# Attention and two feed-forward layers in one kernel: where ScalarE rounds keys and queries, and where VectorE sums, in the first 18 slots

## The reference

```python
scores = scale * np.matmul(q, k.transpose(0, 1, 3, 2))
kth = np.partition(scores, -top_k, axis=-1)[..., -top_k:-top_k + 1]
scores = np.where(scores >= kth, scores, -1000000000.0)
attn = np.exp(scores - np.max(scores, axis=-1, keepdims=True))
attn = attn / (np.sum(attn, axis=-1, keepdims=True) + 1e-09)
x = np.matmul(attn, v)                    # then heads side by side: 2304 x 512
h = x @ w_in                              # layer 1
g = np.where(h >= 1, h, np.where(h <= -1, 0.0, (h + 1) ** 2 / 4.0))
y = g @ w_out
h2 = np.maximum(y @ w_in2, 0.0)           # layer 2
out = h2 * h2 @ w_out2
```

## Time and profile before

| | |
|---|---|
| median of 3 runs | 1221.03 us |
| the profiled execution | 1220.98 us, of which the span from first to last instruction is 1219.2 us |
| mean granted TensorE clock | 0.982 |
| busy | PE 96%, PEld 89%, DVE 68%, ACT 64%, POOL 61% |

### The profile page before, as it was taken

How to read it: one execution, slowest core, us unless ns; L and a number is a source line. 1 busy time by engine, 2 the same in 40 slices (tenths; PEclk the granted TensorE clock), 3 DMA queues, 4 the chain that set the end, 5 groups by cost and what they waited for, 6 DMA issues and landing times.

```text
span 1219.2 us, 22952 instructions
## 1 busy us (share of the span) xinstructions
PE 1174.0 (96%) x8120; PEld 1089.9 (89%) x8120; DVE 833.0 (68%) x1847; ACT 784.0 (64%) x1704; POOL 740.3 (61%) x589
## 2 busy tenths in 40 slices
PE   5878999999999999999999999999999999999998
PEld 3777899999889999999999999998999888998887
DVE  7999999999988799999999987878830211110000
ACT  7887777787656767767676665666554544653343
POOL 6777887888877677677776766666742222222222
PEclk9957999999999999999999999999999999999999
DMA  6777897678869923433458831567449400870000
GB/s 252 266 267 252 282 360 295 251 268 315 302 253 393 379 75 109 147 121 112 140 208 297 294 112 41 130 173 183 109 160 361 167 1 1 338 318 1 1 35 18
DMA packets 93377, 237.34 MB, mean 195 GB/s; under 512 B 10320, under 2 KB 45136, under 8 KB 80976
## 3 DMA queue, kind: packets, MB, share of 16 engines
q1 hardware_dynamic: 93104, 235.62, 54.9%
q10 hardware_dynamic: 160, 0.26, 0.1%
HBM read 164.02 MB, written 71.83 MB: 193 GB/s over the span
## 4 chain that ended last, share of the span: by engine, by line
PE 74%; DVE 9%; POOL 8%; ACT 4%; issue 3%; DMA 1%; SPq 0%; ACTq 0%; POOLq 0%; DVEq 0%
PE h_ps L700 22%; PE y_ps L728 11%; PE y_ps L734 10%; PE pv_ps L659 6%; PE score_ps L700 6%; DVE top L1086 5%; PE tr_ps L632 4%; DVE rest L1088 4%; PE score_ps L605 3%; POOL s_sb L1270 3%; POOL prob L1275 2%; POOL kq_lo L1253 2%; PE y_ps L720 2%; PE y_ps L723 2%; PE tr_ps L720 2%
## 5 line engine op out<-in xcount | busy, mean ns | idle before, releaser
L700 PE MATMUL h_ps<-xt_ks,w_in 128*128 128x256 f32 (+1 forms) x2628 | 384.5, 296 | 2.3 <-ACT rg L961 1.6
L700 PEld LDWEIGHTS h_ps<-xt_ks,w_in 128*128 128x128 f32 x2628 | 342.1, 191 | 12.8 <-ACT rg L961 2.0
L1288 POOL TENSOR_TENSOR g_lo<-rg,g_hi 128x256 fp32r<-128x256 f32 x224 | 169.4, 756 | 270.4 <-ACT g_hi L974 153.6
L1086 DVE MAX8 top<-rest 128x8 f32<-128x576 f32 x432 | 305.1, 746 | 0.4
L1270 POOL TENSOR_SCALAR s_sb<-s_sb,top 128x576 f32<-128x576 f32 x126 | 221.5, 1758 | 31.3 <-DVE top L1086 31.3
L1088 DVE MATCH_REPLACE8 rest<-top,rest 128x576 f32<-128x576 f32 x288 | 211.5, 741 | 0.0
L1275 POOL TENSOR_TENSOR prob<-s_sb,prob 128x576 f32<-128x576 f32 x128 | 182.9, 1431 | 16.3 <-ACT s_sb L856 3.5
L728 PE MATMUL y_ps<-g_hi,w_out 128*128 128x256 f32 x896 | 181.4, 285 | 0.6 <-POOL g_lo L1288 0.5
L734 PE MATMUL y_ps<-w_out,g_hi 128*128 128x512 f32 x448 | 158.5, 395 | 1.0 <-ACT moves L935 0.8
L728 PEld LDWEIGHTS y_ps<-g_hi,w_out 128*128 128x128 f32 x896 | 147.5, 191 | 2.1 <-POOL g_lo L1288 1.0
L659 PE MATMUL pv_ps<-v_sb,pt 128*128 128x65 f32 x1024 | 133.6, 288 | 0.0
(11 more groups left out here) (117 smaller groups left out, 1821.8 us busy)
## 6 DMA issues: line engine op xcount, KB each, us to landing
w_in<-w_scratch SPq DMA_DIRECT2D x32, 1024.0 KB, 7.1
w_out<-w_scratch SPq DMA_DIRECT2D x32, 1024.0 KB, 8.4
xt_ks<-kq_scratch SPq DMA_DIRECT2D x30, 576.0 KB, 7.2
w_scratch<-w_in SPq DMA_DIRECT2D x16, 1024.0 KB, 7.2
w_scratch<-w_out SPq DMA_DIRECT2D x16, 1024.0 KB, 6.7
v_sb<-in_vv_dram SPq DMA_DIRECT2D x48, 325.0 KB, 6.1
qs_g<-kq_scratch SPq DMA_DIRECT2D x120, 128.0 KB, 4.3
moves<-in_w_dram SPq DMA_DIRECT2D x27, 512.0 KB, 5.9
```

Source lines behind the costliest of these rows:

```text
L700: last = pe.matmul(h_bank(k), wi[:, f // 2, w, m, cols], x_part(k, x, m), start=(m == 0 and n == 0), stop=(m == KT - 1 and n == 2))
L1086: dve.max(best, src[:, :]).then_inc(rank_step, 1)
L1288: pool.tensor_tensor(lo_of(k), u_of(k), hi_of(k).bitcast(F32), ALU.subtract).then_inc(g_lo_done, 1)
```

## The change

In slots 1, 3, 5 and 7 ScalarE's rounding of a preparation (`split_new`) goes from ahead of `exponentiate(n, 1)` to behind `copy_shared(n - 1)`, ahead of `split_ahead(n)`. In slots 10, 12, 14 and 16 VectorE's `add_to_total` goes from ahead of `rank(n, 0, 2)` to between the two ranks of op 2, `invert_total` from between these to between the two ranks of op 3, and ScalarE's `scale_pv` from ahead of `copy_scores(n + 1, 0)` to behind `copy_main(n - 1, 0)`. No operation is added or dropped.

```diff
@@ ScalarE, slot(n)
-                if n in SINGLE:
+                if n in SINGLE and n not in PREP_SLOT:
                     scale_pv(n - 2)
                 if nxt:
                     copy_scores(n + 1, 0)
...
                 copy_at(q)
                 if n in PREP_SLOT and n in SINGLE:
+                    scale_pv(n - 2)
                     hi_at(q)
-                if n in SINGLE or q < UP_POS[0]:
+                if n in SINGLE:
                     split_new(n)
                 if here:
                     exponentiate(n, 1)
...
                     copy_shared(n - 1)
                 copy_at(q + 1)
                 hi_at(q + 1)
+                if n < SINGLE[0]:
+                    split_new(n)
                 split_ahead(n)
@@ VectorE, slot(n)
-                    if past and op == 2 + behind and n not in SUMMED:
+                    if past and op == 2 + behind and n not in SUMMED and not (n in SINGLE and n in PREP_SLOT):
                         add_to_total(n - 2)
...
                         rank(n, 0, op)
-                        if op == 2 and n in SINGLE:
+                        if op == 2 and n in SINGLE and n in PREP_SLOT:
+                            add_to_total(n - 2)
+                        if op == (3 if n in PREP_SLOT else 2) and n in SINGLE:
                             invert_total(n - 2)
                         rank(n, 1, op)
```

## The result

| | before | after |
|---|---|---|
| median of the runs side by side, us | 1221.07 (1220.47 to 1224.06, 6 runs) | 1231.26 (1230.34 to 1233.01, 6 runs) |
| profiled execution, us | 1220.98 | 1230.34 |
| its span, us | 1219.2 | 1228.5 |
| VectorE's rank (10, 0) starts, us | 107.25 | 115.62 |
| VectorE's rank (18, 0) starts, us | 193.45 | 202.97 |

The ratio is 1.0082, 95% interval 1.0069 to 1.0096: 8.4 to 11.7 us slower. The forecast was +6.4, with 1230.0 as the top of the range; the medians show +10.2, the two profiled executions +9.3. The direction is right, the size is too small.

A forecast was written before the change was run, and what follows sets the result against it. VectorE's ranking sets the pace up to 107.2 us, and TensorE, busy from 193.4 us, can't absorb early delays. Terms of 6.3 and 0.3 gave +6.6, taken as +6.4: 1227.4 us, range 1222.5 to 1230.0.

The forecast's parts named there:

- Part 1: Rounding (kq_hi) later on ScalarE in slots 1, 3, 5, 7: late masks and loads delay VectorE, growing to +6.3 us.
- T: Start of ScalarE's rounding in slots 1, 3, 5, 7: 27.17, 49.9, 72.7 and 93.4 us.
- T + 6.4: GpSimd: mask(n, 0) can't start earlier than 6.4 us after the rounding's start, behind split_kq and the weight split.
- the steps from T to T: Transposes, scores, copies and times_v between two roundings: 20.7 us with no late load, over VectorE's 19.6 for two slots.
- Slot 9 has no rounding, so it stops there: Slot 9: the delay of VectorE's ranks grows no further than the +6.3 us at rank (9, 1).
- part 2: Sum, reciprocal and scale_pv later in slots 10, 12, 14, 16: slot 10 0, then +0.1 us three times, +0.3.
- The loads: SP's queue: queries of slots 4 and 6 land late, 5.3 us after issue, 0.8 us more delay in slot 3.
- Rival A: Loads of queries land early, so slots 4 and 6 don't wait: rank (9, 1) at 101.6, total 1224.7 us; chance 0.20.
- Rival C: TensorE's clock stays low in slots 8 and 9, 1.6 us a slot: +8 to +8.5, 1229.3 us; chance 0.10.
- after denser work: TensorE: times_v's products take 1.90 us at 98.07, following denser work, against 3.52 at the low clock level.
- That chain had 0.20 us of wait plus some 0.09 of wake-up: ScalarE's chain to g_hi, slot 14: room of 0.3 us against scale_pv's 0.4, so it ends 0.1 us later.
- The sum: Whole kernel: 6.3 + 0.3 = +6.6 us, taken as +6.4, giving 1227.4 us.

The follow-up runs named there:

- the swap: Late rounding in slots 1, 3, 5, 7, plus GpSimd's weight split ahead of the preparation's in slots 0 to 9, against the kernel before: 1220.63 us (-0.7), ratio 0.9994.
- the sum a pair later: Late rounding in slots 1, 3, 5, 7, plus slot 9's sum and reciprocal a pair of ranks later, against the kernel before: 1227.89 us (+6.4), ratio 1.0052.
- slots 3, 5 and 7 late alone: Kernel before with only the rounding of slots 3, 5 and 7 late: 1228.07 us (+6.3), ratio 1.0056.
- part 2 alone: Kernel before with only sum, reciprocal and scale_pv later in slots 10, 12, 14, 16: 1222.49 us (+1.1), ratio 1.0010.
- four pieces: Later sum, reciprocal and scale_pv, with GpSimd's preparation split in four instructions in slots 10, 12, 14, 16, against the kernel before: 1221.94 us (+0.6), ratio 1.0003.
- the rounding's idle place: Changed kernel with weight split first in slots 0 to 9 and rounding behind exponentiate(n, 0) in slots 10 to 16, against before: 1219.24 us (-2.6), ratio 0.9978.
- the two parts alone: Kernel before with only the late rounding of slots 1, 3, 5, 7: 1228.91 us (+7.6); with only the changes in slots 10, 12, 14, 16: 1222.49 us (+1.1).
- only the sum later: Kernel before with only the sum of slots 10, 12, 14, 16 half a pair of ranks later: 1221.91 us (+0.4), ratio 1.0003.
- the two last ones: Changed kernel, weight split first, rounding in ScalarE's idle place in slots 10 to 16: 1219.24 us; the same with slots 1 to 7 rounded early: 1218.64 us.

## Why the prediction was right or wrong

**Part 1's path: right.** Each step of it can be laid beside the profile after:

| | forecast | after |
|---|---|---|
| start T of the rounding, slots 1, 3, 5, 7 | 27.17, 49.9, 72.7, 93.4 | 27.29, 50.01, 73.02, 93.82 |
| mask(1, 0), mask(3, 0) start | 33.55, T + 6.4 = 56.3 | 33.64, 56.36 |
| rank (3, 1) | 39.04 | 39.28 |
| rank (5, 1) | 61.0 | 61.28 |
| rank (7, 1) | 83.8 | 84.29 |
| rank (9, 1) | 104.5 | 105.09 |

The start of the mask at T + 6.4 hit within 0.1 us, and the swap shows that this queue on GpSimd is the cause: with the weight split out of it part 1 costs nothing. How the loss divides between masks and loads is open. Each later rank is 0.2 to 0.6 us behind the forecast, since the steps from T to T were summed slightly short; rank (9, 1) is 6.9 us later than before, not 6.3. (The 49.9 of slot 3 is a slip: 47.6 + 1.4 + 0.8 is 49.8.)

**Part 1's end: "Slot 9 has no rounding, so it stops there" failed.** VectorE's sum reads slot 9's delay too. It waits 1.30 us for the product, and rank (10, 0) is 8.4 us late where I had stopped at 6.3. I had followed only the tiles that the rank reads, and had looked at the product only in part 2's slots. In slots 0 to 8 the sum stands a pair of ranks later in VectorE's order (behind = 2) and is covered; slot 9 is the first of the closer setting, and it receives the whole delay. With the sum a pair later the wait is gone. It also took the clock's low level on that one product, which with slots 3, 5 and 7 late alone was at the high one and made nobody wait.

**The loads: right.** They land late, with 5.4 us from the issue of the second load of queries (62.01 + 0.62) to TensorE's start at 68.05, where the earlier trace rows give 5.3. Rival A, early landing, would have given 101.6 for rank (9, 1). For a transfer of this size the estimate from the Trainium skill, DMA: Bandwidth & Descriptors, "Anatomy of one DMA", is 2.3 us. For these loads, behind six others, the traces don't agree with it.

**Rival C, the clock: its size came out, in part by luck.** I had written +8 to +8.5 for low clock in slots 8 and 9. Rank (10, 0) came at +8.37. Slot 8's product ran at the high level (1.90 us; 3.52 before, at 89.23), slot 9's at the low one (3.52; 1.90 before), and without the second there would have been no wait of 1.30. That is the clock's part; C's sum needs about 2 us of it, and the rest was made up by the steps from T to T. It was the rival nearest to the result, and I had given it 0.10. The rule of the Trainium skill that I cited with it, that the clock follows how busy TensorE has been, is neither borne out nor refuted by these runs. From 60 to 113 us TensorE is busy 39.28 us at a clock of 0.56 in after and 42.91 us at 0.63 before, which would agree. But "after denser work" was a misreading: in the 7 us ahead of the short product at 98.07 TensorE was busy 5.75 us with 27 matmuls, in the 7 ahead of the long one at 79.24 it was busy 6.27 with 26. And the same program up to slot 9's sum had its high level on slot 8's product in two kernels' executions and on slot 7's in a third.

**Part 2: "That chain had 0.20 us of wait plus some 0.09 of wake-up" failed.** The direction is right, and so is the first step (scale_pv's time leaves an idle place of ScalarE and comes ahead of the rounding). The size was 0.1 for a pair and is 0.38 to 0.43, and the path behind the rounding was another. I took the idle time in front of g_hi, 0.20 us, for room of ScalarE against an activate that stays where it is. It doesn't stay: the rounding moves by 0.38, GpSimd's split with it, and the activate doesn't end before the split has. Both sides of the wait moved together, and so it is 0.20 in before, in part 2 alone and in after alike. So the chain runs rounding, split, activate, VectorE's next rank, and was closed all along; g_hi, at which I had looked, only follows it: with four pieces it waits for nothing, in the rounding's idle place 0.48 us, and the pair goes by neither. The waits for the product, 0.34 to 0.38 us, lay ahead of the activate, and what their removal frees the activate spends again, which is why it alone brings nothing.

**The sum.** In the profiled execution: slots 0 to 9 +8.37, slots 10 and 11 -0.02 (rank (12, 0) from 129.25 to 137.60), three pairs +1.17, from slot 18 on -0.2: +9.3 of span. Forecast were 6.3, 0, 0.3 and 0. Against the sum of 6.6 that is 2.7 more: 1.30 for the product, 0.63 for the steps from T to T and 0.14 up to rank (10, 0) in part 1, 0.87 in part 2, less 0.2 behind slot 18; and 0.2 more that I had taken off for the loads. The medians are 0.8 us further apart than the profiled executions, and the medians of the two parts alone sum to +8.7 instead of +10.2; the interval, 8.4 to 11.7, allows both, and what the rest is stays open. The range was too narrow: I had bounded each cost of part 2 by -0.37 and +0.4 a pair, and yet let C's price end the range without adding part 2's upper bound to it: 8.5 + 1.2 = 9.7 gives 1230.7, above the profiled execution of after though still below its median.

## What to carry to other kernels

Before moving a step to where its engine has time, list what each later queue does behind it; here an engine idled 5 us and then did three things in a row, and swapping two of them took back all that the move had cost. A delay doesn't stop where its cause stops: look for the next consumer with a closer setting. Where an instruction is longer than its peers in the profile of before (0.46 against 0.41 us), see what runs on the neighbouring engine and whether the two end together, because then the chain is closed there though no wait is shown. Where an engine is busy all of a stretch, its busy time itself has to be read, not only its waits.

## What the runs showed of the hardware that I had not expected

VectorE's scalar_tensor_tensor on two 128x256 tiles of SBUF, 0.41 us in most slots, lasts up to 1.26 us while GpSimd's two-input tensor_tensor on 128x1216 runs, and ends 0.27 to 0.28 us after that has ended, in the kernels before and after, in part 2 alone, with only the sum later and in the two last ones, such as 139.96 and 140.24 before, 148.69 and 148.97 after. No wait is shown; it is in the busy time. With the GpSimd instruction in four pieces VectorE gets in between two of them. The Trainium skill, GPSIMD Engine Reference, "8. Key points", says that GpSimd "Shares its SBUF interfaces with VectorE — contention with DVE instructions in a 2-port perf mode or with two SBUF inputs"; the traces agree, with the numbers above. Before has one more such row, beside GpSimd's mask at 198.53 (1.43 us):

```profile
199.04 1.19 DVE L1149 SCALAR_TENSOR_TENSOR rg<-rg 128x256 f32<-128x256 f32 x1
```

The length of one and the same product changed between 1.90 and 3.52 us, TensorE's high and low level, from slot to slot and, over the same instructions, between two kernels' executions. That moved a product by 1.6 us and a rank by 1.2 us, half as much as some of the effects looked for here. The granted clock shown ahead of its first fall in a trace didn't tell these apart: it reads 1.00 over products of both lengths.
